# Attention scores from q and k turned in 32x32 blocks by VectorE instead of by TensorE, one core

## The reference

```python
# q, k, v: 4 x 8 x 768 x 64
scores = q @ k.T / 8
keep = (key < 4) | ((0 <= query - key) & (query - key < 128))
a = softmax(where(keep, scores, -1e9))
x = (a @ v).transpose(0, 2, 1, 3).reshape(3072, 512)
h = ((x @ w1) * (x @ w2)) @ w3
x = h @ w_out
logits = x @ w_gate + bias[modality]
e = argmax(logits)
out = softmax(logits)[e] * (relu(x @ ew1[e]) @ ew2[e])
```

## Time and profile before

| | us |
|---|---|
| median of 3 runs (936.12 to 936.34) | 936.24 |
| the profiled execution | 936.7 |
| its span, first to last instruction | 935.1 |
| TensorE busy in it | 915.5 |
| VectorE busy | 561.2 |
| ScalarE busy | 394.2 |
| POOL busy | 179.0 |

### The profile page before, as it was taken

The page is one execution under the profiler, slowest core; times in us unless marked ns, Lnnn a source line. Parts: engine busy times, 40 slices in busy tenths (PEclk is TensorE's granted clock), DMA queues, the critical chain, the costliest instruction groups (busy, mean ns, idle before and its releaser), DMA issues.

```text
span 935.1 us, 19775 instructions
## 1 busy us (share of the span) xinstructions
PE 915.5 (98%) x6994; PEld 852.6 (91%) x6994; DVE 561.2 (60%) x1373; ACT 394.2 (42%) x953; POOL 179.0 (19%) x289
## 2 busy tenths in 40 slices
PE   7999999999999999999999999999999999999995
PEld 5778899999999999999999999999999999999994
DVE  6876564574565574564575563257566666666655
ACT  3556343442352442343443341251455555555553
POOL 2441112231222231231230231002100000000000
PEclk9999999999999999999999999999999999999998
DMA  7646413222222222222222202044611116111111
GB/s 223 195 139 215 154 53 94 63 74 68 57 81 78 68 69 69 68 69 77 68 68 69 69 34 74 19 181 150 240 45 44 48 44 226 45 47 45 45 45 40
DMA packets 108973, 83.22 MB, mean 89 GB/s; under 512 B 85343, under 2 KB 85343, under 8 KB 108896
## 3 DMA queue, kind: packets, MB, share of 16 engines
q1 hardware_dynamic: 104368, 68.53, 25.2%
q0 software_dynamic: 4240, 13.66, 3.8%
q10 hardware_dynamic: 288, 0.00, 0.0%
HBM read 56.70 MB, written 25.74 MB: 88 GB/s over the span
## 4 chain that ended last, share of the span: by engine, by line
PE 90%; DVE 3%; issue 2%; POOL 1%; ACT 1%; DMA 1%; DVEq 0%; ACTq 0%; SPq 0%; POOLq 0%
PE acc_a L321 6%; PE acc_b L321 6%; PE acc_b L323 6%; PE acc_b L322 6%; PE acc_a L322 5%; PE acc_a L323 5%; PE attn L942 4%; PE misc L315 4%; PE misc L316 4%; PE misc L317 4%; PE acc_a L315 3%; PE acc_b L315 2%; PE attn L317 2%; PE attn L316 2%; PE acc_b L316 2%; PE acc_b L317 2%
## 5 line engine op out<-in xcount | busy, mean ns | idle before, releaser
L779 POOL TENSOR_TENSOR probs<-scores,row_inv 128x256 f32<-128x256 f32 x96 | 67.3, 723 | 247.8 <-DVE row_inv L1806 247.8
L1316 ACT ACTIVATE ew<-raw_e 128x1024 fp32r (+1 forms) x100 | 101.3, 1051 | 14.1 <-issue 14.1
L321 PE MATMUL acc_a<-xT_w,w 128*128 128x384 f32 x256 | 90.2, 352 | 0.0
L321 PE MATMUL acc_b<-xT_w,w 128*128 128x384 f32 x256 | 89.1, 348 | 0.7 <-DVE ab L1850 0.7
L323 PE MATMUL acc_b<-xT_w,w 128*128 128x384 f32 x256 | 86.5, 338 | 0.0
L322 PE MATMUL acc_a<-xT_w,w 128*128 128x384 f32 x256 | 86.5, 338 | 0.0
L322 PE MATMUL acc_b<-xT_w,w 128*128 128x384 f32 x256 | 86.5, 338 | 0.0
L323 PE MATMUL acc_a<-xT_w,w 128*128 128x384 f32 x256 | 86.5, 338 | 0.0
L1850 DVE TENSOR_TENSOR ab<-acc_b,ab 128x384 f32<-128x384 f32 x64 | 35.5, 555 | 81.2 <-PE acc_b L323 80.7
L1337 ACT ACTIVATE scores<-scores,neg_max 128x136 f32<-128x136 f32 x192 | 75.6, 397 | 7.3 <-DVE neg_max L1796 7.3
L1940 DVE TENSOR_TENSOR ew<-raw_e,ew 128x1024 fp32r<-128x1024 f32 x52 | 60.4, 1220 | 28.7 <-ACT ew L1316 28.7
(11 more groups left out here) (354 smaller groups left out, 2788.7 us busy)
## 6 DMA issues: line engine op xcount, KB each, us to landing
raw_e<-in_moe_w SPq DMA_DIRECT2D x24, 512.0 KB, 7.0
raw<-in_moe_w SPq DMA_DIRECT2D x16, 512.0 KB, 6.1
x_in<-routed SPq DMA_DIRECT2D x29, 257.0 KB, 3.0
q_nat<-in_q SPq DMA_DIRECT2D x24, 256.0 KB, 3.2
k_nat<-in_k SPq DMA_DIRECT2D x24, 256.0 KB, 4.0
v_nat<-in_v SPq DMA_DIRECT2D x24, 256.0 KB, 4.4
x_mid<-x_out SPq DMA_DIRECT2D x24, 256.0 KB, 2.0
x_in<-x_mid SPq DMA_DIRECT2D x24, 256.0 KB, 2.7
```

What stands on the lines that cost most here:

```text
L321: pe.matmul(o, w_hi, x_hi, start=start, stop=False, skip_group_check=True)
L779: pool.tensor_tensor(probs[:, at, side * HALF:(side + 1) * HALF], scores[:, at, side, SINKS:], row_inv[:, at].unsqueeze(2).broadcast_to([P ...
L1316: return act.activation(o, i, ACT.Copy)
```

## The change

q and k are loaded in quarters: quarter `part` (32 partitions) of `q_nat` holds two heads, four successive tokens of a head beside each other on a partition, 1024 bytes in a piece (`quarter_of`, `quarter_in`); that makes eight loads of 64 KB per tile instead of two of 256 KB. VectorE turns square blocks of 32x32 in each quarter (`turn_qk`, four instructions per tile: two for k into `keys`, two for q into `qT`), so that a head lies on 32 partitions in two halves of 32 features (index `e`). ScalarE scales `qT` in place (`scale_q`). The scores of a head and a query half are now two products of 32 rows that add up in PSUM; the four quarters write to the four banks. TensorE's transposes, ScalarE's copies out of PSUM and the hand-over of `left` and `right` between transposes and probabilities are gone. `turn_qk` of a tile stands on VectorE behind `take_probsT` of the tile before. Three semaphores for tables become one, `known`; their uses keep their places.

```diff
+        qk_turned, q_ready = sem("qk_turned"), sem("q_ready")
...
+        def heads_of(part):
+            first = 4 * (part // 2) + part % 2
+            return slice(first, first + 3, 2)
+
+        def quarter_of(x, part):
+            return x[32 * part:32 * part + 32, :].rearrange("j (a m) -> j a m", a=2)
+
+        def quarter_in(x, b, i, part):
+            return x[b, heads_of(part), i * P:(i + 1) * P, :].rearrange("a (j f) d -> j a (f d)", f=4)
+
         @block.sync
         def _(sp):
             sp.sem_inc(g_stored, 1)
             def load_qk(t):
-                sp.wait_ge(right_full, 2 * t.no - 1)
-                sp.dma_start(heads(q_nat[:, :]), rows(q, t.b, t.i)).then_inc(qk_in, 16)
-                sp.dma_start(heads(k_nat[:, :]), rows(k, t.b, t.i)).then_inc(qk_in, 16)
+                if t.no >= 1:
+                    sp.wait_ge(qk_turned, 4 * t.no)
+                for part in range(4):
+                    sp.dma_start(quarter_of(q_nat, part), quarter_in(q, t.b, t.i, part)).then_inc(qk_in, 16)
+                for part in range(4):
+                    sp.dma_start(quarter_of(k_nat, part), quarter_in(k, t.b, t.i, part)).then_inc(qk_in, 16)
...
-            sp.dma_start(heads(q_nat[:, :]), rows(q, 0, 0)).then_inc(qk_in, 16)
-            sp.dma_start(heads(k_nat[:, :]), rows(k, 0, 0)).then_inc(qk_in, 16)
+            load_qk(tiles[0])
...
             def carry_keys(t):
 
-                pool.wait_ge(right_empty, 2 * t.no + 1)
+                pool.wait_ge(qk_turned, 4 * t.no + 2)
+                if t.no >= 1:
+                    pool.wait_ge(scores_full, 4 * t.no)
                 own = keys[:, t.par, :, 2:5:2, SINKS:]
...
-            def attn_transposes(t):
-
-                pe.wait_ge(qk_in, 32 * t.no + 32)
-                pe.wait_ge(left_empty, 2 * t.no)
-                for c in range(PAIRS):
-                    mm = pe.transpose(left[:, c * P:(c + 1) * P], q_nat[:, c * P:(c + 1) * P], ident[:, :])
-                mm.then_inc(left_full, 1)
-                pe.wait_ge(right_empty, 2 * t.no)
-                for c in range(PAIRS):
-                    mm = pe.transpose(right[:, c * P:(c + 1) * P], k_nat[:, c * P:(c + 1) * P], ident[:, :])
-                mm.then_inc(right_full, 1)
-
             def attn_scores(t):
 
-                pe.wait_ge(left_empty, 2 * t.no + 1)
-                pe.wait_ge(right_empty, 2 * t.no + 1)
+                pe.wait_ge(q_ready, t.no + 1)
+                pe.wait_ge(qk_turned, 4 * t.no + 2)
+                pe.wait_ge(left_empty, t.no)
+                pe.wait_ge(right_empty, t.no)
                 pe.wait_ge(k_sink_ready, t.b + 1)
                 pe.wait_ge(k_carried, (QB - 1) * t.b + t.i)
                 pe.wait_ge(scores_read, 2 * t.no)
-                for g in range(2):
-                    for odd in range(2):
-                        r = D * odd
-                        for h in (4 * g + odd, 4 * g + 2 + odd):
-                            at = (h % 4) // 2 * 3 * BLK
+                for a in range(2):
+                    at = a * 3 * BLK
+                    for e in range(2):
+                        for part in range(4):
+                            r, o = 32 * part, sbank[part // 2][part % 2]
                             for half in range(2):
                                 q0 = half * HALF
-                                mm = pe.matmul(sbank[g][odd][q0:q0 + HALF, at:at + 3 * BLK], qT[r:r + D, h // 2, q0:q0 + HALF],
-                                               keys[r:r + D, t.par, h // 2, 2 * half:2 * half + 3, :].rearrange("p a n -> p (a n)"),
-                                               start=True, stop=True)
-                        mm.then_inc(scores_full, 1)
+                                mm = pe.matmul(o[q0:q0 + HALF, at:at + 3 * BLK], qT[r:r + 32, 2 * a + e, q0:q0 + HALF],
+                                               keys[r:r + 32, t.par, 2 * a + e, 2 * half:2 * half + 3, :]
+                                               .rearrange("p a n -> p (a n)"), start=e == 0, stop=e == 1, skip_group_check=True)
+                            if (a, e) == (1, 1):
+                                mm.then_inc(scores_full, 1)
...
-                    pe.wait_ge(empty, 2 * t.no + 1)
...
-            attn_transposes(t[0])
...
-            attn_transposes(t[1])
...
-                attn_transposes(tb)
...
-                attn_transposes(tc)
...
-                    attn_transposes(group_tile(g + 2, 0))
...
-            def take_q(t):
-                act.wait_ge(left_full, 2 * t.no + 1)
-                act.activation(qT[:, :, :], left[:, :].rearrange("p (c n) -> p c n", c=PAIRS), ACT.Copy, scale=SCALE)\
-                    .then_inc(left_empty, 1)
-
-            def take_k(t):
-                act.wait_ge(right_full, 2 * t.no + 1)
-                if isinstance(t.no, int) and t.no == 0:
-                    act.wait_ge(zeroed, 1)
-                copy(keys[:, t.par, :, 2:5:2, SINKS:], right[:, :].rearrange("p (c a n) -> p c a n", c=PAIRS, a=2))\
-                    .then_inc(right_empty, 1)
+            def scale_q(t):
+                act.wait_ge(qk_turned, 4 * t.no + 4)
+                act.activation(qT[:, :, :], qT[:, :, :], ACT.Copy, scale=SCALE).then_inc(q_ready, 1)
...
-                take_q(tb)
-                take_k(tb)
+                scale_q(tb)
...
+            def turn_qk(t):
+
+                ve.wait_ge(qk_in, 128 * t.no + 128)
+                if t.no == 0:
+                    ve.wait_ge(zeroed, 1)
+                else:
+                    ve.wait_ge(scores_full, 4 * t.no)
+                for a in range(2):
+                    ve.transpose(keys[:, t.par, 2 * a:2 * a + 2, 2:5:2, SINKS:].rearrange("p e m (j f) -> p e f m j", f=4),
+                                 k_nat[:, a * 256:(a + 1) * 256].rearrange("p (f e n) -> p e f n", f=4, e=2)).then_inc(qk_turned, 1)
+                for a in range(2):
+                    ve.transpose(qT[:, 2 * a:2 * a + 2, :].rearrange("p e (j f) -> p e f j", f=4),
+                                 q_nat[:, a * 256:(a + 1) * 256].rearrange("p (f e n) -> p e f n", f=4, e=2)).then_inc(qk_turned, 1)
...
-                ve.wait_ge(right_empty, 2 * t.no + 1)
+                ve.wait_ge(qk_turned, 4 * t.no + 2)
...
             t = [Tile(n // QB, n % QB) for n in range(TILES)]
+            turn_qk(t[0])
             take_k_sinks(t[0], 0)
...
             take_probsT(t[0], 1)
+            turn_qk(t[1])
             gate_weights(1)
...
                 take_probsT(ta, 1)
+                turn_qk(tb)
                 mlp_u(g, 2)
...
                 take_probsT(tb, 1)
+                turn_qk(tc)
                 if g == GROUPS - 2:
...
+                if after:
+                    turn_qk(after)
```

More of the change, by code:

```diff
@@ L697, in _ @@
                 load_tile(2, tile)
-            sp.wait_ge(weights_known, 1)
-            sp.wait_ge(units_known, 1)
+            sp.wait_ge(known, WEIGHTS)
+            sp.wait_ge(known, JOBS_KNOWN)
             n_pairs = sp.value_load(units_i[0:1, 0:1], min_val=PAIRED, max_val=MOST_PAIRS)
@@ L897, in attn_scores @@
                 pe.wait_ge(scores_read, 2 * t.no)
-                for g in range(2):
-                    for odd in range(2):
-                        r = D * odd
-                        for h in (4 * g + odd, 4 * g + 2 + odd):
-                            at = (h % 4) // 2 * 3 * BLK
+                for a in range(2):
[3 more added lines that the diff above has]
+                            r, o = 32 * part, sbank[part // 2][part % 2]
                             for half in range(2):
                                 q0 = half * HALF
-                                mm = pe.matmul(sbank[g][odd][q0:q0 + HALF, at:at + 3 * BLK], qT[r:r + D, h // 2, q0:q0 + HALF],
-                                               keys[r:r + D, t.par, h // 2, 2 * half:2 * half + 3, :].rearrange("p a n -> p (a n)"),
-                                               start=True, stop=True)
-                        mm.then_inc(scores_full, 1)
+                                mm = pe.matmul(o[q0:q0 + HALF, at:at + 3 * BLK], qT[r:r + 32, 2 * a + e, q0:q0 + HALF],
[3 more added lines that the diff above has]
+                                mm.then_inc(scores_full, 1)
             def attn_probsT(t):
                 pe.wait_ge(scores_read, 2 * t.no + 2)
-                for part, (o, full, empty) in enumerate(((left, left_full, left_empty), (right, right_full, right_empty))):
+                for part, (o, full) in enumerate(((left, left_full), (right, right_full))):
                     pe.wait_ge(probs_normal, 4 * t.no + 2 * part + 2)
-                    pe.wait_ge(empty, 2 * t.no + 1)
                     for hh in range(4):
@@ L927, in attn_values @@
                 i = t.i
-                pe.wait_ge(left_empty, 2 * t.no + 2)
-                pe.wait_ge(right_empty, 2 * t.no + 2)
+                pe.wait_ge(left_empty, t.no + 1)
+                pe.wait_ge(right_empty, t.no + 1)
```

(22 more changed lines are left out.)

26 lines of the change are left out of this document (12 added, 14 removed).

## The result

The changed kernel takes **931.34 us** (median of 4 runs, 929.98 to 931.55); the kernel before, run beside it, 936.29. The ratio is 0.9943, with a 95% interval of 0.9926 to 0.996. So it is faster by 5 us, inside the range, but the forecast was 923.0: of 13 us of gain less than half came. The profiled execution took 931.45 us, with a span of 929.8.

What follows compares the result with a forecast made beforehand. TensorE was taken to bound the middle stretch (busy 418.81 of 420.00 us). 936.7 - 17.6 + 2.2 + 2.1 = 923.4, put at 923 for the median; forecast 918 to 928, range 916 to 938.

Steps and rivals of the forecast that it cites:

- Eight transposes off TensorE: TensorE, each tile: removing the transposes saves 0.88 us in each of 20 middle tiles, 17.6 us in all.
- Scores unchanged: TensorE, each tile's scores: 64 records over eight places still take eight rounds of 0.17 us, so 1.6 us and no change.
- A: Rival, scores: only four places work at once, so 16 rounds, 33 us more, 956 us; chance 0.12.
- B: Rival, scores: weight loads set the round, 0.22 us instead of 0.17, 8.7 us more, 932 us; chance 0.12.
- D: Rival, scores: matmuls run in strict order, 25 rounds more per tile, 103 us more, 1026 us; chance 0.02.
- First half of the scores later: First tile of each group from the second: masks start later, delaying TensorE's acc_b 0.36 us in six groups, +2.2 us.
- A transpose at 0.42 us: VectorE, four added transposes per tile: 0.42 us each, 1.6 us for four; bounds 0.3 and 0.84 us.
- the slack of 0.4 between tb and tc: Middle, second to third tile of a group: q scaled at 338.75, TensorE asks at 339.18, so no wait.
- Rival C: VectorE's transposes take twice as long, or POOL's carrying slows them: 937 us, no change; chance 0.13, spread over 928 to 942.
- The opening, +2.1: Before about 88 us: VectorE is the late engine, so its added transposes delay TensorE, a net loss of 2.1 us.
- edits at no cost: SyncE's eight loads per tile, POOL's earlier carrying of keys and ScalarE's one copy fewer were taken to cost nothing.
- 1.3 us at block 4: Opening, tile 1: transposes push the masks to about 43.9, so TensorE's block 4 of w3 waits until some 45.6, +1.3.

## Why the prediction was right or wrong

- **Eight transposes off TensorE, 17.6 us: right.** 14.5 us came between tiles 3 and 23. The missing 3.1 are the 2.2 of the next point, the wait for q between tb and tc (0.16 in each of three groups, 0.5), and 0.7 between tiles 3 and 4, where the stop at acc_b grew from 0.69 to 1.22 us; the forecast counted the later masks only from the second group on.
- **Scores unchanged: right.** 1.30 us from first to last start; rivals A (2.6), B (1.7) and D are out. But the reason was wider than the truth: I had it that the places run side by side whatever the order of issue, and with the row group outermost they don't. The program happened to have the order that works.
- **First half of the scores later, +2.2: right.** By the starts of the scores it cost 0.33 to 0.40 us in each of the six groups, where 0.36 was forecast.
- **A transpose at 0.42 us: too small.** 0.63. I had named the 16 bytes as the upper end of the range and taken the lower middle. In the middle stretch this used up the slack of 0.4 between tb and tc, and cost 0.5 us in all; that it cost no more is luck. Rival C, which wanted 0.84, gave 8 us for it there and did not come; had it come, the kernel with q turned twice shows 7.7 us for nearly the same length.
- **The opening, +2.1: this step failed, at +8.9.** The failing sentence stands among the edits at no cost: "POOL's carrying of keys starts earlier, behind k". It was true and it was not free. I moved VectorE's list in time and never laid POOL's list, moved as well, beside it. Taking POOL's split away gives back 5.4 us, taking the biases away 5.9, and taking the biases away in the kernel before nothing. What remains is 3.6 us at tile 3's scores in the kernel with the split later (91.77 against 88.19), where the forecast had 2.1. Its trace says where: 1.3 us at block 4, as forecast; 0.3 at tile 2's scores and 0.5 at tile 2's values, which wait 0.74 us for VectorE's sink step, where the forecast had a gain of 0.1 for both; 1.5 at the last fold product, where it had 1.3. The 0.4 us that tile 0 was to gain did not come. Which of this the longer transposes cause was not tested by itself.
- The warning was in the trace of before. Ahead of the row at 38.49, VectorE's fold split of the block before takes 2.79 us. Its twin of the same form, at 39.67, took 0.68. Beside the slow one POOL's subtraction for w1 ran, from 35.05 to 37.42:

```profile
35.17 2.79 DVE L1837 TENSOR_TENSOR w_fold<-row_out,w_fold 128x512 fp32r<-128x512 f32 x1
```

A smaller sign of the same kind stands ahead of 42.45:

```profile
41.18 0.77 DVE L1752 TENSOR_TENSOR bias_t<-mod_not,bias_b 128x192 f32<-128x192 f32 x1
```

Its twin of the same form, at 40.90, took 0.36 us, and POOL's copies of keys (41.02 to 42.21) ran beside the slow one. A duration of two or four times that of its twin is a reason to look at what the neighbour on SBUF does at that moment.

The sum with what the traces show: 936.7 - 17.6 + 2.2 + 0.5 + 0.7 + 8.9 = 931.4, the profiled execution took 931.45. The last three terms are read from that execution itself, so this closes the account and forecasts nothing. That the time came out beside rival B's 932 is chance: a round of the scores took 0.17 us, not its 0.22.

## What to carry to other kernels

When work moves to VectorE, draw the new times of POOL's list beside VectorE's, not of VectorE's alone: a tiny operation on SBUF operands can be held for the whole of a POOL operation, and both lists move. Put such operations where POOL works on nothing large, or let POOL's be the ones that wait. And price a stop of TensorE with what its clock may do afterwards: the one of 4.33 us brought some 2.6 us more, and one idle of 1.51 us brought over 1 us more in two traces and nothing in eight.

## What the runs showed of the hardware that I had not expected

- **VectorE held by POOL.** Operations on 24 numbers took 1.01, 2.23 and 2.35 us beside POOL's cast and subtraction and 0.17 to 0.18 without them, and each ended within 0.04 us of POOL's operation. The masks, with one operand in PSUM, kept 0.43 to 0.44 us beside the same subtraction. It goes the other way too: POOL's cast, 1.03 us elsewhere, took 1.53 while VectorE's fold split was running. The Trainium skill (SBUF — State Buffer, section Who interferes with whom) states this: VectorE and GpSimd share a pair of ports. VectorE needs it for copies, casts and operations with a scalar in the modes that use two ports, and for operations with two inputs in SBUF beside a GpSimd operation that reads SBUF; the one that issues first keeps it for its whole instruction and the other fully blocks. The trace agrees, with the ends above, and so it does for the masks, which have one input in SBUF; in which mode an operation ran, no trace shows. By that rule the loss could have been forecast.
- **Steps between the numbers of a transpose.** 0.63 us for 256 numbers per partition with them, 0.68 us for 512 without.
- **TensorE passes waiting matmuls, but few.** When s_odd first starts, six of s_even's eight records still wait in the kernel before, and the last six of sixteen with the row group outermost, though all were issued ahead of it.
- **The clock behind a stop.** At block 4, from start to start, the granted clock fell to 0.50 behind the stop of 4.33 us and stayed at 1.00 behind those of 3.26 us (the turnings moved), 1.42 and 0.68 us. The length of the stop alone does not decide it: the idle of 1.51 us before tile 1's values is in ten traces of the changed kernel and its variants; in two of them (the biases later; POOL's split later with u ahead) the clock fell to 0.50 behind it, and in eight it stayed at 1.00. What makes the difference stays open.
